# Turning of output quarters moved from the end of a second-MLP run to the gate of that run's fourth product

## What is computed

```python
for t in range(S):
    state = gamma * state + einsum('bhd,bhe->bhde', k[:, :, t], v[:, :, t])
    y[:, :, t] = scale * einsum('bhd,bhde->bhe', q[:, :, t], state)
x = y.transpose(0, 2, 1, 3).reshape(B * S, H * D)          # 3072 x 512
h = maximum(x @ w_in, 0.0)
x = h * h @ w_out
xn = x / sqrt(mean(x * x, -1) + 1e-6) * rms_g
g, val = xn @ w_gate, xn @ w_val
out = (g / (1 + exp(-g)) * val) @ w_out2
```

## Time and profile before

| | before |
|---|---|
| median of 3 runs | 1085.37 us (1085.33 to 1085.92) |
| the profiled execution | 1085.6 us |
| its span, first to last instruction | 1083.8 us |
| PE, DVE, ACT, POOL busy, of the span | 99%, 83%, 56%, 31% |
| TensorE's granted clock | 1.000 of full |

### The profile page before, as it was taken

How to read it: one execution, slowest core, us unless ns; L and a number is a source line. 1 busy time by engine, 2 the same in 40 slices (tenths; PEclk the granted TensorE clock), 3 DMA queues, 4 the chain that set the end, 5 groups by cost and what they waited for, 6 DMA issues and landing times.

```text
span 1083.8 us, 15742 instructions
## 1 busy us (share of the span) xinstructions
PE 1068.7 (99%) x5988; PEld 893.7 (82%) x5988; DVE 894.9 (83%) x946; ACT 601.7 (56%) x902; POOL 338.9 (31%) x240
## 2 busy tenths in 40 slices
PE   8999999999999999999999999999999999999998
PEld 8888788888888888888888887888777788777898
DVE  4686999878989879889899988877887986878684
ACT  5886565466644666554665545655444555544453
POOL 0764552004450005430035553005445003554000
PEclk9999999999999999999999999999999999999999
DMA  9999548763447644366642326631224761130455
GB/s 354 381 406 406 215 183 283 234 212 117 176 154 245 218 144 162 146 245 196 226 143 84 135 99 235 211 115 62 59 76 147 262 195 40 46 111 20 136 185 185
DMA packets 80970, 196.46 MB, mean 181 GB/s; under 512 B 24448, under 2 KB 34688, under 8 KB 76032
## 3 DMA queue, kind: packets, MB, share of 16 engines
q1 hardware_dynamic: 78448, 191.24, 51.2%
q10 hardware_dynamic: 2448, 4.22, 1.0%
HBM read 152.87 MB, written 42.48 MB: 180 GB/s over the span
## 4 chain that ended last, share of the span: by engine, by line
PE 83%; DVE 6%; ACT 4%; DMA 3%; issue 2%; POOL 1%; ACTq 0%; SPq 0%; DVEq 0%; POOLq 0%
PE Y L809 12%; PE Y L811 12%; PE Y L810 12%; PE X L809 8%; PE X L810 8%; PE X L811 8%; PE Z L809 7%; PE Z L810 7%; PE Z L811 7%; DMA item_scratch<-ops 2%; PE Z L768 1%; PE Z L758 1%; ACT k_dec L925 1%; ACT gt L1036 1%; DVE hid L1624 1%
## 5 line engine op out<-in xcount | busy, mean ns | idle before, releaser
L670 POOL TENSOR_TENSOR w_ops<-raw_w,w_ops 128x512 fp32r<-128x512 f32 x90 | 129.0, 1434 | 512.7 <-ACT w_ops L937 512.6
L997 ACT CAST ops<-hid 128x1024 fp32r<-128x1024 f32 x147 | 154.8, 1053 | 160.7 <-PE Z L811 53.9
L1346 DVE TENSOR_TENSOR ops<-hid,ops 128x1024 fp32r<-128x1024 f32 x147 | 179.6, 1222 | 46.2 <-ACT ops L997 46.1
L670 POOL TENSOR_TENSOR w_ops<-sums_w,w_ops 128x512 fp32r<-128x512 f32 x120 | 175.4, 1465 | 115.2 <-ACT w_ops L937 114.7
L809 PE MATMUL Y<-ops,w_ops 128*128 128x512 f32 x360 | 141.3, 392 | 6.2 <-ACT Y L1004 4.9
L811 PE MATMUL Y<-ops,w_ops 128*128 128x512 f32 x360 | 140.2, 390 | 0.0
L810 PE MATMUL Y<-ops,w_ops 128*128 128x512 f32 x360 | 140.1, 389 | 0.0
L1036 ACT ACTIVATE gt<-gt 128x512 f32<-128x512 f32 x72 | 45.4, 633 | 138.2 <-DVE gt L1605 41.0
L809 PE MATMUL Y<-ops 128*128 128x512 f32 (+1 forms) x288 | 104.4, 362 | 0.0
L810 PE MATMUL Y<-ops 128*128 128x512 f32 (+1 forms) x288 | 104.4, 362 | 0.0
L811 PE MATMUL Y<-ops 128*128 128x512 f32 (+1 forms) x288 | 104.4, 362 | 0.0
(11 more groups left out here) (164 smaller groups left out, 2348.5 us busy)
## 6 DMA issues: line engine op xcount, KB each, us to landing
ops<-item_scratch SPq DMA_DIRECT2D x147, 512.0 KB, 3.8
raw_w<-w_f SPq DMA_DIRECT2D x30, 1024.0 KB, 4.9
item_scratch<-hid SPq DMA_DIRECT2D x30, 512.0 KB, 3.1
qk_sb<-qkv SPq DMA_DIRECT2D x24, 512.0 KB, 8.5
kv_sb<-qkv SPq DMA_DIRECT2D x20, 512.0 KB, 8.9
y_scratch<-hid SPq DMA_DIRECT2D x12, 512.0 KB, 5.4
raw<-y_scratch SPq DMA_DIRECT2D x3, 2048.0 KB, 9.6
raw<-w_b SPq DMA_DIRECT2D x5, 1024.0 KB, 5.3
```

Source lines behind the costliest of these rows:

```text
L670: nc.gpsimd.tensor_tensor(w_ops[:, k, 1], front_w_source(m, k), f32(w_ops[:, k, 0]), ALU.subtract).then_inc(w_lo, 1)
L997: nc.scalar.copy(hop_at(n)[:, 0], hid[:, 2 * g:2 * g + 2, OPERAND[k], :]).then_inc(hop_hi, 1)
L1346: nc.vector.tensor_tensor(hop[:, 1], hid[:, 2 * g:2 * g + 2, OPERAND[k], :], f32(hop[:, 0]), ALU.subtract).then_inc(hop_lo, 1)
```

## The change

The two halves of `turn` become two functions. The transposes stand ahead of `gate_x`, the scaling right behind it, in the same runs q = 1 to 4 of tiles 1 and 2; the end of the run has none of it. The instructions, their shapes and their places in memory are the same. The wait for the norm's factors goes with the scaling, those for the quarter's data with the transposes. ACT's, PE's, POOL's and SP's programs are unchanged.

```diff
                 if fresh:
                     dve.wait_ge(rinv_b_loaded, 16 * (t + 1))
+                if t and 1 <= q <= 4:
+                    turn(t - 1, q - 1)
                 gate_x(run, m)
+                if t and 1 <= q <= 4:
+                    scale_turned(t - 1, q - 1)
                 prep(m, 4, fresh, TILES + t)
                 if not fresh:
                     value_x(run, q)
...
-                if t and 1 <= q <= 4:
-                    turn(t - 1, q - 1)
                 if bk:
                     low_hop(bk, 1)
...
             def turn(t, i):
-                s = (A, Dd, Bb, C)[i]
...
+                s, flat, place = turn_places(i)
+                rows = flat.rearrange("p (b f i) -> p b f i", b=16, f=2)
                 if s == A:
                     dve.wait_ge(x_taken, run_b2(t) + 1)
-                    dve.wait_ge(rinv_t_loaded[t], 64)
                 if s == C:
                     dve.wait_ge(y_taken, run_b2(t) + 1)
                 for f in range(2):
-                    op = nc.vector.transpose(turned_rows[:, :, f, :], place[:, N * f:N * f + N])
+                    op = nc.vector.transpose(rows[:, :, f, :], place[:, N * f:N * f + N])
                 op.then_inc(turned, 1)
+
+            def scale_turned(t, i):
+                s, flat, place = turn_places(i)
+                n = s % 2
+                if s == A:
+                    dve.wait_ge(rinv_t_loaded[t], 64)
                 dve.wait_ge(turned, 4 * t + i + 1)
...
                 nc.vector.tensor_tensor(place.rearrange("p (k s d) -> p k s d", k=4, s=4),
-                                        flat.rearrange("p z n -> p (z n)").rearrange("p (k s d) -> p k s d", k=4, s=4),
+                                        flat.rearrange("p (k s d) -> p k s d", k=4, s=4),
                                         by_block.to_broadcast([P, 4, 4, 64]), ALU.mult).then_inc(turn_scaled, 1)
```

More of the change, by code:

```diff
@@ L1607, in front2_run, with turn_places @@
                     mean_square(TILES - 1)
-                if t and 1 <= q <= 4:
-                    turn(t - 1, q - 1)
                 if bk:
                     low_hop(bk, 1)
+            def turn_places(i):
+                s = (A, Dd, Bb, C)[i]
+                flat = hid[:, 5, 0:2, :].rearrange("p z n -> p (z n)")
+                return s, flat, out_sb[:, s].rearrange("p t d -> p (t d)")
             def turn(t, i):
-                s = (A, Dd, Bb, C)[i]
-                flat, place = hid[:, 5, 0:2, :], out_sb[:, s].rearrange("p t d -> p (t d)")
-                turned_rows = flat.rearrange("p z n -> p (z n)").rearrange("p (b f i) -> p b f i", b=16, f=2)
+                s, flat, place = turn_places(i)
+                rows = flat.rearrange("p (b f i) -> p b f i", b=16, f=2)
                 if s == A:
                     dve.wait_ge(x_taken, run_b2(t) + 1)
-                    dve.wait_ge(rinv_t_loaded[t], 64)
                 if s == C:
@@ L1623, in turn @@
                 for f in range(2):
-                    op = nc.vector.transpose(turned_rows[:, :, f, :], place[:, N * f:N * f + N])
+                    op = nc.vector.transpose(rows[:, :, f, :], place[:, N * f:N * f + N])
                 op.then_inc(turned, 1)
+            def scale_turned(t, i):
[3 more added lines that the diff above has]
+                    dve.wait_ge(rinv_t_loaded[t], 64)
                 dve.wait_ge(turned, 4 * t + i + 1)
-                n = s % 2
                 by_block = rinv_turn[:, t, :, 4 * n:4 * n + 4].rearrange("p s k -> p k s").unsqueeze(3)
                 nc.vector.tensor_tensor(place.rearrange("p (k s d) -> p k s d", k=4, s=4),
-                                        flat.rearrange("p z n -> p (z n)").rearrange("p (k s d) -> p k s d", k=4, s=4),
+                                        flat.rearrange("p (k s d) -> p k s d", k=4, s=4),
                                         by_block.to_broadcast([P, 4, 4, 64]), ALU.mult).then_inc(turn_scaled, 1)
```

## The result

The median went from 1085.68 to 1078.30 us (six runs each), a ratio of 0.9934 with a 95% interval of 0.9921 to 0.9946: 7.4 us faster, as forecast. The profiled execution of the changed kernel took 1079.18 us with a span of 1077.4. That is 1.0 more than the 1076.4 that the sum gives, and the whole of it lies ahead of anything the change touches: the second MLP's first product begins at 554.12 us in place of 553.05. In the first 20 us of the span the granted clock was 0.91 of full in this execution and 1.00 in that of the kernel before.

What follows compares the result with a forecast made beforehand. PE, busy 99% of the span, was taken as the bound. Eight runs gain 0.927 us each and all other terms cost nothing: 1085.37 - 7.4 = 1078.0 us, range 1076.9 to 1080.8.

Steps and rivals of the forecast that it cites:

- the sum: Whole kernel: 8 x 0.927 = 7.4 us off the profiled span of 1083.8 us, giving 1076.4.
- The gain: Second MLP, runs behind a turn: each of eight runs gets 0.927 us shorter, 7.4 us in all.
- The cause: End of a run: the turn holds DVE's queue 2.39 us, delaying the tail, ACT's copy into Y and PE's product 2.
- What is late next: Copy into Y after the change: it waits for product 0 instead of the tail, and is 1.2 us early.
- Ahead of the gate: Transposes' new place: DVE idles there waiting for product 3, so the pair of 1.22 to 1.3 us costs nothing.
- The hole: DVE's idle time before the gate, waiting for product 3: 2.7 us in the new order, 1.45 us in q = 1.
- the bound of -1.0: Sums ahead of the gate: change in us if a 1.66 us sum shrinks to 0.68; claimed to stay inside the idle time.
- the bound of +1.0: Sums ahead of the gate: the opposite limit, in us, on their change in duration; claimed to stay inside the idle time.
- Behind the gate: Scaling's new place, between gate and value: 1.23 us against 0.70 idle, fits by 0.11; cost 0, bounds 0 to 4.2 us.
- the remaining cover ahead of product 6: Between DVE's L1587 and PE's product 6: 1.25 us of delay that PE would not notice.
- POOL: Its operations on the next weights: the scaling, 795.5 to 796.7, fits between them, ending at 795.0 and starting from 796.8.
- The item: First item of tile 1's back run: PE's 0.75 us wait likely goes, but Z waits for DVE's low part; gain nothing.

Runs made afterwards that it cites:

- the halves: Two variants of the changed kernel, with only the scaling or only the transposes back at the end of a run: 1077.88 us (0.9921) and 1080.15 us (0.9939).

## Why the prediction was right

*The gain.* 7.42 us were worked out from the windows, the traces show the eight runs at 19.04 us, and the medians fell by 7.38. The step from PE's waits (4.9 us in total) to what they cost (7.4) was needed: the waits alone give two thirds.

*The cause.* That the turn's place at the end of the run held PE, and the copy into Y was what passed it on, is shown by the halves and by the doubled transposes: nothing up to the spare time, then one for one, 1.21 us for 1.21, as far as the clock stayed at full.

*What is late next.* Product 0 for the copy, as said. The spare time was put at 1.2 us and is 1.5: the prediction let product 0 land 0.5 us behind the place where product 1 starts, and the copy began 0.20 behind it (767.74, against 764.82 + 2.72 = 767.54). The 789.02 that the prediction has for product 2 without the stall is 0.15 early: in the trace the run began at 783.73, and two products take 5.44, so of the 0.93 us 0.78 lies ahead of that product's first matmul and 0.15 in the matmuls behind it. The forecast does not hang on it.

*Ahead of the gate.* The hole was put at 2.7 us, which is 1.4 to 1.5 left behind the transposes. Left were 2.53. The term that was off is the sums: I had kept L1400 at 1.66 us, and it fell to 0.69, at the bound of -1.0 that stood beside it. POOL's operations had moved against it. Before, one of them lay across L1400's start at 792.85; after, the next one began only as L1400 ended:

```profile
792.23 1.73 POOL L670 TENSOR_TENSOR w_ops<-sums_w,w_ops 128x512 fp32r<-128x512 f32 x1
```

```profile
772.07 1.30 POOL L670 TENSOR_TENSOR w_ops<-sums_w,w_ops 128x512 fp32r<-128x512 f32 x1 [1.19 <-ACT w_ops L937]
```

The forecast did not hang on it: six of the eight holes had room for either bound. In q = 1, where L1400 stayed at 1.66, the bound of +1.0 was not inside the hole, as the prediction has it; there only the cover behind the gate would have been left. The transposes began at 772.07 too and took 1.30 us, as they do before (784.27, with no POOL operation beside them), so these two did not hold each other up, as said. In q = 1 the hole was as small as forecast, with 0.24 us left where the trace of before gave 0.15 to 0.23.

*Behind the gate.* It fitted. The value came 0.35 us later behind its gate, not 0.53, since consecutive instructions overlap. That the remaining cover ahead of product 6 is real is shown by the turn put wholly ahead of the gate and wholly behind it.

*POOL.* No meeting in the changed kernel: the scaling takes 1.22 us, and it ends at 777.73 with POOL's next operation from 777.85. The 0.12 us between them were forecast at 0.1. How near it is, the experiments show: a scaling 1.3 us later ties with POOL and loses in two of eight runs.

*The item.* Nothing won, nothing lost, as said, and for the reason given: the low part ahead of Z. That the item would now land in time was less sure than it sounded. It did in the changed kernel, but with the scaling at the end of the run or all of the turn ahead of the gate PE waited 0.3 and 0.9 us for it. Its group of transfers was issued in the same order there, but later: the group's first load (L413) stands 4.4 us ahead of product 3 in the changed kernel, and 3.2 and 3.4 us ahead in these two. In the experiments in which it stood 3.5 us ahead or more, PE did not wait. What sets the length of the wait was not settled: it is not in the order of these figures.

## What to carry to other kernels

A step that ends the queue of one stage stands ahead of the next stage's first step, and that may be the one that frees a buffer. Look for the place in the same queue where the engine waits anyway, and measure two things there: the idle time, and how late the step behind it may be before the bounding engine notices. Then ask what else runs at the new place; in the changed kernel 0.12 us kept two engines from meeting.

## What was not expected of the hardware

A wait of PE of 1.80 us was followed by a fall of the granted clock to 0.50 in four runs of eight, strictly every second one, and cost 1.6 us more each time. Waits of 0.62 us in the kernel before and of 1.65 in the kernel with three scalings had no such fall in any of eight. So a run with this wait took 2.1 us above its 19.04 where the clock stayed, and 3.7 where it fell. Why it fell in every second run no experiment shows.

Engines meet at more than semaphores. DVE's scaling and POOL's operation, with no wait between them, gave way to whichever began first, down to 0.01 us: 2.31 against 1.22 us for the same scaling, 2.37 against 1.29 for POOL's. The transposes beside POOL's operation showed no such thing: both began at 772.07 and took 1.30 us.
